# Two-phase feed-forward kernel with chunked attention: q and k of the first eight pairs loaded in 256-byte runs and turned on TensorE

## The reference

```python
scores = q_c @ k_c.T / 8 ; attn = softmax(scores) ; x = attn @ v_c      # per head and 64-row chunk
x = rows of 8 heads x 64 = 512 ; xn = x / rms(x) * rms_g
h = silu(xn @ w_gate) * (xn @ w_val)                                     # 512 -> 1536
y = h @ w_out                                                            # 1536 -> 512
u = y @ w_in2 ; g = u * relu6(u + 3) / 6 ; out = g @ w_out2              # 512 -> 2048 -> 512
```

## Time and profile before

| | |
|---|---|
| median of 3 runs (lowest to highest) | 1726.42 us (1720.36 to 1731.27) |
| profiled execution: time, span | 1721.54 us, 1719.7 us |
| TensorE busy, mean granted clock | 1653.0 us (96%), 0.979 |
| VectorE, ScalarE, GpSimd busy | 1047.3, 869.6, 753.0 us |
| transposed probabilities of pair 6; first product of A | 56.9; 61.51 us |
| first product of phases B, C, D | 711.55, 980.93, 1337.92 us |
| idle of TensorE before products at 874.25 (B), 1028.60 (C) | 0.78, 1.30 us |

### The profile page before, as it was taken

How to read it: one execution, slowest core, us unless ns; L and a number is a source line. 1 busy time by engine, 2 the same in 40 slices (tenths; PEclk the granted TensorE clock), 3 DMA queues, 4 the chain that set the end, 5 groups by cost and what they waited for, 6 DMA issues and landing times.

```text
span 1719.7 us, 29694 instructions
## 1 busy us (share of the span) xinstructions
PE 1653.0 (96%) x11325; PEld 1606.1 (93%) x11330; DVE 1047.3 (61%) x1413; ACT 869.6 (51%) x1361; POOL 753.0 (44%) x711
## 2 busy tenths in 40 slices
PE   6898999999999999999999999999999999999996
PEld 4787988999999999999999999999999999999996
DVE  3877778767755555565554786665666855444442
ACT  3556666664544444454444555554555643433441
POOL 6443434437786665411220467777775510110011
PEclk6899999999999999999999999999999999999998
DMA  9675667635466555788889866557649966666672
GB/s 156 135 183 140 162 156 177 162 106 177 150 234 210 200 201 187 273 284 291 307 305 326 290 232 220 207 182 257 224 169 312 385 212 196 208 216 203 203 219 74
DMA packets 340509, 366.87 MB, mean 213 GB/s; under 512 B 196112, under 2 KB 305424, under 8 KB 337168
## 3 DMA queue, kind: packets, MB, share of 16 engines
q1 hardware_dynamic: 327184, 330.10, 60.9%
q0 software_dynamic: 8832, 34.35, 6.2%
q10 hardware_dynamic: 4352, 0.53, 0.2%
HBM read 200.80 MB, written 164.10 MB: 212 GB/s over the span
## 4 chain that ended last, share of the span: by engine, by line
PE 76%; DVE 4%; DMA 3%; issue 3%; ACT 2%; POOL 2%; DVEq 0%; POOLq 0%; ACTq 0%; SPq 0%
PE bx L861 12%; PE by L861 12%; PE by L863 12%; PE by L862 12%; PE bx L863 12%; PE bx L862 12%; DMA hl_b<-h_scratch 2%; PE att L803 1%; DVE tx L1372 1%; PE att L831 1%; PE att L906 1%; DMA h_scratch<-ht 1%; PE att L840 1%; DMA wr<-wd_scratch 1%; DVE vb L1415 0%
## 5 line engine op out<-in xcount | busy, mean ns | idle before, releaser
L861 PE MATMUL bx<-tx,wr 128*128 128x384 f32 x840 | 287.8, 343 | 9.0 <-ACT gb L1053 3.9
L861 PE MATMUL by<-tx,wr 128*128 128x384 f32 x840 | 288.4, 343 | 5.2 <-DVE ub L1394 4.6
L863 PE MATMUL by<-tx,wr 128*128 128x384 f32 x840 | 282.1, 336 | 0.0
L862 PE MATMUL by<-tx,wr 128*128 128x384 f32 x840 | 281.9, 336 | 0.0
L863 PE MATMUL bx<-tx,wr 128*128 128x384 f32 x840 | 281.8, 335 | 0.0
L862 PE MATMUL bx<-tx,wr 128*128 128x384 f32 x840 | 281.7, 335 | 0.0
L1420 DVE TENSOR_TENSOR hl_d<-hl_d 128x1536 fp32r<-128x1536 f32 x84 | 146.5, 1776 | 88.4 <-ACT hl_d L1129 88.4
L1420 DVE TENSOR_TENSOR hl_b<-hl_b 128x1152 fp32r<-128x1152 f32 x84 | 118.1, 1421 | 106.1 <-ACT hl_b L1129 105.4
L1723 POOL DMA_DIRECT2D out_dram<-row x72 | 37.6, 528 | 309.0 <-ACT row L1171 301.1
L861 PEld LDWEIGHTS bx<-tx,wr 128*128 128x128 f32 x840 | 158.4, 189 | 13.7 <-issue 4.2
L861 PEld LDWEIGHTS by<-tx,wr 128*128 128x128 f32 x840 | 158.5, 189 | 10.8 <-DVE ub L1394 3.7
(11 more groups left out here) (164 smaller groups left out, 3845.1 us busy)
## 6 DMA issues: line engine op xcount, KB each, us to landing
hl_d<-u_scratch SPq DMA_DIRECT2D x84, 768.0 KB, 4.4
hl_b<-h_scratch SPq DMA_DIRECT2D x84, 576.0 KB, 5.5
u_scratch<-ut SPq DMA_DIRECT2D x48, 576.0 KB, 3.6
h_scratch<-ht SPq DMA_DIRECT2D x36, 576.0 KB, 3.7
u_scratch<-ub SPq DMA_DIRECT2D x96, 192.0 KB, 2.9
u_scratch<-ub SPq DMA_DIRECT2D x48, 384.0 KB, 2.9
h_scratch<-vb SPq DMA_DIRECT2D x72, 192.0 KB, 3.3
h_scratch<-vb SPq DMA_DIRECT2D x36, 384.0 KB, 3.3
```

Source lines behind the costliest of these rows:

```text
L861: pe.matmul(dst, w_hi, m_hi, start=start, stop=False, skip_group_check=not opens)
L862: pe.matmul(dst, w_hi, m_lo, start=False, stop=False, skip_group_check=not opens)
L863: return pe.matmul(dst, w_lo, m_hi, start=False, stop=stop, skip_group_check=not opens)
```

## The change

It has three parts.

1. q and k of pairs 0 to 7 are loaded as they lie, in 256-byte runs (one head of one row), two DMAs of 128 KB each for q and for k of a pair: q on SP, k of pairs 0 to 3 on ScalarE's queue, the others on SP. TensorE turns them (`turn_qk`, eight 128x128 transposes of a pair into the bank pair in which the pair's scores will lie), VectorE copies q out (`copy_q`), ScalarE k (`copy_k`). The later pairs stay as they were. The dummy products are placed anew (24, 4 and 4 instead of 18, 2 and one a pair), and GpSimd waits for k of pair 0 before the first load of v and for k of pair 1 before the first raw weights. The weight work of ScalarE and GpSimd in the prologue moves to later pairs; `sums(2)` comes last.
2. The normed rows have two buffers (`xn`, `xn_b`), so that scaling pair n waits for the transposes of pair n-2, no longer n-1.
3. The splits in place, the weight blocks and the units are placed anew: the first half of phase B is split one slot group later and the third moves into phase B; of the splits of phase C one moves to slots 0 and 2 of step 42 and the others to slots 7 and 9, and 9 and 12; block 4 is loaded before GpSimd's last sums of phase A, blocks 5 and 6 wait for one and two products of phase B; unit 22 moves into phase B, and the units there come every 2.5 products instead of every 3.

The core of the diff, without its context lines:

```diff
@@ -108,10 +108,11 @@
-    FIRST_PAIRS = (range(0, 1), range(1, 2), range(2, 4), range(4, 6), range(6, 8))
-    qk_first = [at(f"qk_first{i}", [P, 2, len(FIRST_PAIRS[i]) * D], F32, U0 + (8192, 12288, 16384, 24576, 32768)[i]) for i in range(5)]
+    NQ = 8
+    qk_first = at("qk_first", [P, NQ, 2, D], F32, U0 + 8192)
+    xn_b = at("xn_b", [P, D + 1], F32, U0 + 67584)

@@ -183,8 +184,10 @@
-    q_loaded_first = [sem(f"q_loaded_first{i}") for i in range(5)]
-    k_loaded_first = [sem(f"k_loaded_first{i}") for i in range(5)]
+    q_loaded_first = [sem(f"q_loaded_first{n}") for n in range(NQ)]
+    k_loaded_first = [sem(f"k_loaded_first{n}") for n in range(NQ)]
+    q_turned = sem("q_turned")
+    k_turned = sem("k_turned")

@@ -449,7 +448,7 @@
-    RAW_AT = {6: (14, 9), 7: (14, 10), 8: (16, 11), 9: (16, 13), 10: (18, 11), 11: (18, 13), 12: (19, 12), 13: (20, 2), 23: (34, 13)}
+    RAW_AT = {6: (14, 9), 7: (14, 10), 8: (16, 11), 9: (16, 13), 10: (18, 11), 11: (18, 13), 12: (19, 12), 13: (20, 2), 22: (34, 0)}

@@ -459,7 +458,7 @@
-    U_B = 22
+    U_B = 21

@@ -476,15 +475,15 @@
-        return [u for u in range(U_B + 1, UEND) if 3 * (u - U_B) + after == g]
-    SPLIT_AT = {(0, 0): ((34, 8), (34, 9)), (0, 1): ((34, 10), (34, 11)), (0, 2): ((35, 9), (35, 10)),
-                (0, 3): ((36, 0), (36, 0)), (0, 4): ((36, 1), (36, 1)), (0, 5): ((36, 2), (36, 2)), (0, 6): ((36, 3), (36, 3)),
+        return [u for u in range(U_B + 1, UEND) if 5 * (u - U_B) // 2 + after == g]
+    SPLIT_AT = {(0, 0): ((34, 7), (34, 9)), (0, 1): ((34, 9), (34, 11)), (0, 2): ((35, 7), (35, 9)),
+                (0, 3): ((36, 0), (36, 0)), (0, 4): ((36, 2), (36, 2)), (0, 5): ((36, 3), (36, 3)), (0, 6): ((36, 4), (36, 4)),
-                (1, 2): ((42, 8), (42, 9)), (1, 3): ((42, 10), (42, 11)), (1, 4): ((43, 8), (43, 9)), (1, 5): ((43, 10), (43, 11)),
-                (1, 6): ((44, 8), (44, 9)), (1, 7): ((44, 10), (44, 11)),
-                (2, 0): ((63, 8), (63, 9)), (2, 1): ((64, 8), (64, 9)), (2, 2): ((66, 0), (66, 0)), (2, 3): ((66, 1), (66, 1)),
+                (1, 2): ((42, 0), (42, 2)), (1, 3): ((42, 7), (42, 9)), (1, 4): ((42, 9), (42, 12)), (1, 5): ((43, 7), (43, 9)),
+                (1, 6): ((43, 9), (43, 12)), (1, 7): ((44, 7), (44, 9)),
+                (2, 0): ((63, 7), (63, 9)), (2, 1): ((64, 7), (64, 9)), (2, 2): ((66, 0), (66, 0)), (2, 3): ((66, 1), (66, 1)),

@@ -514,16 +513,12 @@
-        def load_first(i, src, which, loaded):
-            t, p = tp_of(FIRST_PAIRS[i].start)
-            pairs = len(FIRST_PAIRS[i])
-            for piece in range(8):
-                g, b = piece // 2, piece % 2
-                e, hf = g // 2, g % 2
-                by_parity = src[2 * p:2 * (p + pairs)].rearrange("c (j e) (n t) d -> e n t (c j) d", e=2, t=TB)
-                sp.dma_start(qk_first[i][g * TB:(g + 1) * TB, which, :].rearrange("t (m b d) -> t b m d", b=CH // TB, d=TB)[:, b],
-                             by_parity[e, t * (CH // TB) + b][:, :, hf * TB:(hf + 1) * TB]).then_inc(loaded[i], 16)
+        def load_first(n, src, which, loaded):
+            t, p = tp_of(n)
+            for c in range(2):
+                sp.dma_start(qk_first[c * CH:(c + 1) * CH, n, which, :].rearrange("t (h d) -> t h d", d=DH),
+                             src[2 * p + c, :, t * CH:(t + 1) * CH, :].rearrange("h t d -> t h d")).then_inc(loaded[n], 16)

@@ -657,10 +652,10 @@
-        for i in range(5):
-            load_first(i, q, 0, q_loaded_first)
-            if i > 1:
-                load_first(i, k, 1, k_loaded_first)
+        for n in range(NQ):
+            load_first(n, q, 0, q_loaded_first)
+            if n > 3:
+                load_first(n, k, 1, k_loaded_first)

@@ -779,6 +774,14 @@
+    def rows_at(n):
+        return xn_b if n < NG and n % 2 == 1 else xn
+    def turn_bank(n):
+        return bx[:, 0:2] if n % 2 == 1 else att[:, SB:SB + 2]

@@ -804,10 +807,24 @@
+        def turn_qk(n):
+            if n == 0:
+                pe.wait_ge(consts_ready, 2)
+            if n > 1:
+                pe.wait_ge(probsT_copied, n - 1)
+            for i, loaded, done in ((0, q_loaded_first, q_turned), (1, k_loaded_first, k_turned)):
+                pe.wait_ge(loaded[n], 32)
+                by_batch = turn_bank(n)[:, i, :].rearrange("p (c j t) -> p j c t", c=2, j=HJ)
+                for j in range(HJ):
+                    tr = pe.transpose(by_batch[:, j], qk_first[:, n, i, j * P:(j + 1) * P], ident[:, :])
+                tr.then_inc(done, 1)
-                pe.wait_ge(consts_ready, 6)
+                pe.wait_ge(consts_ready, 7)

@@ -864,6 +881,9 @@
+            if m == 0 and st == 0 and o < 2:
+                pe.wait_ge(*((q_transposed, NQ), (k_transposed, NQ))[o])

@@ -912,22 +932,20 @@
-        keep_busy(18)
+        keep_busy(24)
+        turn_qk(0)
+        keep_busy(4)
-        keep_busy(2)
+        turn_qk(1)
+        keep_busy(4)
-            if n < 2 or n == S_FIRST - 1:
+            if n < S_FIRST:
+                scores(n + 1)
+                turn_qk(n + 2)
-                keep_busy(1)
-                scores(n + 1)
-            elif n < S_FIRST:
-                scores(n + 1)
-                attend(n)
-                keep_busy(1)

@@ -978,16 +996,17 @@
-        def load_first_k(i):
-            t, p = tp_of(FIRST_PAIRS[i].start)
-            pairs = len(FIRST_PAIRS[i])
-            for piece in range(8):
-                g, b = piece // 2, piece % 2
-                e, hf = g // 2, g % 2
-                by_parity = k[2 * p:2 * (p + pairs)].rearrange("c (j e) (n t) d -> e n t (c j) d", e=2, t=TB)
-                act.dma_start(qk_first[i][g * TB:(g + 1) * TB, 1, :].rearrange("t (m b d) -> t b m d", b=CH // TB, d=TB)[:, b],
-                              by_parity[e, t * (CH // TB) + b][:, :, hf * TB:(hf + 1) * TB]).then_inc(k_loaded_first[i], 16)
+        def load_first_k(n):
+            t, p = tp_of(n)
+            for c in range(2):
+                act.dma_start(qk_first[c * CH:(c + 1) * CH, n, 1, :].rearrange("t (h d) -> t h d", d=DH),
+                              k[2 * p + c, :, t * CH:(t + 1) * CH, :].rearrange("h t d -> t h d")).then_inc(k_loaded_first[n], 16)
+        def copy_k(n):
+            act.wait_ge(k_turned, n + 1)
+            act.activation(qkT[:, 1, :], turn_bank(n)[:, 1, :], ACT.Copy).then_inc(k_transposed, 1)

@@ -1171,23 +1190,24 @@
-        load_first_k(0)
-        load_first_k(1)
-        act.wait_ge(consts_ready, 6)
+        for n in range(4):
+            load_first_k(n)
+        act.wait_ge(consts_ready, 7)
+        copy_k(0)
+            copy_k(n + 1)
-            if n == 0:
-                weight_hi(0, 0)
-                weight_hi(0, 1)
-                weight_hi(1, n - 2)
+                weight_hi(0, n - 2)
+            if n in (4, 5):
+                weight_hi(1, n - 4)

@@ -1233,9 +1253,8 @@
-                if m == B0 - 1 and slot in (7, 10, 13):
-                    hh = (7, 10, 13).index(slot)
-                    half_hi(0, 0, hh // 2, hh % 2)
+                if m == B0 - 1 and slot in (9, 12):
+                    half_hi(0, 0, 0, (9, 12).index(slot))

@@ -1245,6 +1264,7 @@
+                    half_hi(0, 0, 1, 0)

@@ -1330,6 +1350,11 @@
+        def copy_q(n):
+            dve.wait_ge(q_turned, n + 1)
+            dve.tensor_copy(qkT[:, 0, :], turn_bank(n)[:, 0, :]).then_inc(q_transposed, 1)

@@ -1344,9 +1369,9 @@
-            if n > 0:
-                dve.wait_ge(x_transposed, n)
-            dve.tensor_tensor(by_parity(xn[:, 0:D]), o[:, :, :, 0:DH], row_recip[:, :, :].unsqueeze(3).to_broadcast([P, 2, HJ, DH]), ALU.mult).then_inc(attn_scaled, 1)
+            if n > 1:
+                dve.wait_ge(x_transposed, n - 1 if n <= NG else n)
+            dve.tensor_tensor(by_parity(rows_at(n)[:, 0:D]), o[:, :, :, 0:DH], row_recip[:, :, :].unsqueeze(3).to_broadcast([P, 2, HJ, DH]), ALU.mult).then_inc(attn_scaled, 1)

@@ -1454,16 +1479,13 @@
-        transpose_qk(0)
+        copy_q(0)
-            if n % 2 == 1 or n == S_FIRST:
-                scale_attention(n - 1)
-            transpose_qk(n + 1)
+            copy_q(n + 1)
-            if n in (2, 4):
+            if n > 0:

@@ -1517,9 +1539,8 @@
-                if m == B0 - 1 and slot in (8, 11, 13):
-                    hh = (8, 11, 13).index(slot)
-                    half_lo(0, 0, hh // 2, hh % 2)
+                if m == B0 - 1 and slot in (11, 13):
+                    half_lo(0, 0, 0, (11, 13).index(slot))

@@ -1530,6 +1551,7 @@
+                    half_lo(0, 0, 1, 0)

@@ -1723,39 +1745,41 @@
-        load_raw(0)
-        for const, value in ((half[:, :], 0.5), (minus_half[:, :], -0.5), (xn[:, D:D + 1], (EPS_RMS * D) ** 0.5)):
+        for const, value in ((half[:, :], 0.5), (minus_half[:, :], -0.5), (xn[:, D:D + 1], (EPS_RMS * D) ** 0.5), (xn_b[:, D:D + 1], (EPS_RMS * D) ** 0.5)):
+        pool.wait_ge(k_loaded_first[0], 32)
+        pool.wait_ge(k_loaded_first[1], 32)
+        load_raw(0)
+        load_first_v(1)
```

(35 more changed lines are left out.)

## The result

The changed kernel takes 1712.1 us (median of 11 runs, 1708.2 to 1720.8) where the kernel before takes 1723.6 beside it: a ratio of 0.9937, 95% interval 0.9918 to 0.9956, so 10.9 us (8 to 14) are gained where 26 were forecast. A second set of runs (`after_b`) gave 0.9942 (0.9919 to 0.9964). The profiled execution took 1711.4 us, span 1709.6, 10.1 less than the span before, and it splits by the first product of each phase. "Mark" is the product right behind the x transposes of pair 6, the tenth of phase A, at which TensorE has done the same work in all kernels.

The account below looks back on a forecast made before the run. Loads in 128-byte packets and half-clock TensorE were taken to bound the prologue. Gains 14 (prologue) + 3 (step 0) + 8.4 (passage) + 1.7 (C) - 1 (B) = 26.1 us gave 1700 us against the median 1726.4, range 1688 to 1718.

Parts of the forecast that it names:

- the likeliest case: Whole kernel: the forecast as it stands, 1694 to 1705 us, chance 0.47.
- Passage, B and C: Phase changes: passage from A to B gains 4.2 and 4.2 us, C gains 1.7, B is charged 1.
- The next late thing: Phase B: load of half 6, held on SP by stores of the sums, is late next, about 6 us earlier than now.
- The slower case: Phase B becomes bound by transfers through SP's wait before each of 12 raw loads: 1735 us, chance 0.05.
- the pace of the loop and its start: Prologue: scores 0 at about 10.6, probabilities of pairs 0 and 1 at 14.6 and 18.6, then 4.8 us a pair.
- loads stop being the bound: Prologue: a pair's q and k need 2.2 us of the engines, less than half of a pair's time.
- the term for the work between the pairs: Prologue: GpSimd's weight work between the powers adds 1 us in all.
- they cost nothing: Prologue: the two waits added on GpSimd cost nothing unless k lands after 8 us.
- I take the full clock: Prologue: TensorE stays at full clock, idling some 0.7 of 4.8 us a pair; the half-clock rival, 1722 us, had 0.14.
- step 0: First step of phase A: gains 3 of the 4.2 us lost to half clock, bounds 0 and 4.2.
- half of it arrives: Rival: clock falls for a third of the prologue, powers wait longer, or landing binds the passage; 1705 to 1712, chance 0.28.
- the loads stay the bound: Rival, prologue: 256-byte packets at 17.5 ns, 7 pairs at 6 us, first product at 56; 1708 us, chance 0.06.

Follow-up runs that it names:

- p_tables: Kernel before with only the new places of splits, weight blocks, units and first halves at the phase changes; prologue as before: 1712.2 us, 0.9946 of the kernel before.
- n_gate: m_dum with the raw weights of unit 0 behind the first power too, weight work a pair later, ScalarE's unit 1 parts behind the last norm: 1710.7 us, 0.9941.
- f_fill: Changed kernel with VectorE's split of the first operand behind the last early pair's scores instead of ahead: 0.9943 of the kernel before.
- g3: g2 with the last early pair's power and norm ahead of unit 2's weight load, GpSimd's split and ScalarE's early operand part: 0.9942 of the kernel before.
- m_dum: m_all with dummy products: 8 ahead of pair 3's turn, 2 a pair, 12 at the end: 1707.8 us, 0.9920, and again 1706.5 us, 0.9922.
- c_clock: Changed kernel with added dummies only: 18 ahead of pair 3's turn, 2 a pair, 12 ahead of the sixth's and the last x transposes: 1709.4 us, 0.9920.
- g2: n_gate with unit 0's raw weights loaded once q of pair 3 is there, sums and splits a pair earlier: 0.9924 of the kernel before.
- g2_nod: g2 without dummies except those of the start: 0.9953 of the kernel before; 1717.2 us against g2's 1712.3 on one chip.
- t_dum: p_tables with dummies in TensorE's idle time of the prologue, q and k still by VectorE in 128-byte runs: 0.9951 of the kernel before.
- s_sums2: Changed kernel with GpSimd's sums of unit 2 ahead of the early x sums instead of behind all x sums: 0.9942 of the kernel before.
- p_prologue: Changed kernel with the phase changes' tables, blocks and halves as before, so only the prologue's part: 1719.0 us, 0.9984 of the kernel before.
- m_all: Changed kernel with two GpSimd loads behind powers, unit 1 sums later, first operand's split behind the scores, unit 2 parts three slots later: 1708.1 us, 0.9935.
- l_pure: Changed kernel with two GpSimd loads (unit 1 raw weights, third group's v, 1 MB) issued behind the first power: 0.9945 of the kernel before.
- after: The changed kernel itself, first set of runs and its profile: 1712.1 us, 0.9937 of the kernel before.
- l_loads: l_pure with GpSimd's and ScalarE's weight work also moved to later pairs: 0.9955 of the kernel before.

## Why the prediction was right and wrong

The time lies in the range (1712 in 1688 to 1718), but the gain is less than half of the forecast's, and the likeliest case was not the one that came. By the 1% bound it is "within 1%", which had 0.25.

*Right: the phase changes.* Passage, B and C were given 9.1 us together (8.4 and 1.7 less 1); `p_tables` measured 9.3 (6 to 13), and the profile shows 4.1, 2.6 and 2.2 by phase, less 1.8 in D. The places are less sure than the sum: `p_tables` has 3.2, 1.6, 2.2 and -0.3 there. The next late thing was the half held on SP, as named. The slower case, raw loads in phase B, did not show: its largest wait after the passage is 0.88.

*Right: the pace of the loop and its start.* Scores 0, pair 0 and pair 1 came within 0.8 us of the forecast; a pair takes 4.61 at full clock where nothing is late, and `n_gate` ran pairs 3 to 6 near that pace.

*Wrong: "loads stop being the bound".* This is the step that failed for the first product. It compared q and k's 2.2 us of the engines a pair with the pair's time and left out GpSimd's 2.5 MB, which now all go out between 6.4 and 15.2 us (v of the second and third groups of pairs went at 22.5 and 29.1 before, at 10.4 and 13.5 after). That made q of pair 3 late by 4.26 us and, with the clock, pair 2's probabilities by some 5.5. I had priced the packets from stretches in which nothing else moved, and not asked who shares the engines. With fewer loads ahead of it, q lands some 3 us sooner (`n_gate`).

*Wrong: the term for the work between the pairs.* The other 4 us of the 9.4 by which the first product was late stand ahead of pairs 5 and 6. For GpSimd's weight work I had added 1 us, but 18.6 and five pairs of 4.8 are 42.6, so the sum does not hold it; its sums of unit 1 cost 1.34 at one place. VectorE's split of the first operand was in no term: it is the 2.69 ahead of pair 6 (`f_fill`: 0.34 with it moved).

*Wrong: "they cost nothing"*, of the two waits added on GpSimd. k of pair 1 landed at 8.85, past the 8 us that I had set, and TensorE waited 0.92 us for the first v at 17.47. Queued behind the waits are not only v and the norms, which I named, but the raw weights, and behind those GpSimd's sums and splits of two units and the x sums. With the loads early, q is late; with the loads late (`n_gate`, `g3`), that line is late. With first products at 48.91 and 50.58, near the forecast's, the marks of these two are 75.38 and 76.08, and their totals are the changed kernel's. That this step takes the rest of the gain is argued from these rows and not shown: no run takes the two waits out, and `m_dum`, with unit 0's raw weights where the changed kernel has them, has no wait on the second operand and its mark at 72.3. The forecast ended its count at the first product; once that is early, the prologue ends with the second operand.

*Wrong by size: the clock.* "I take the full clock" held where TensorE was not waiting, so the reasoning on the loop was right; the waits above brought half clock for 7 us in one profile of the changed kernel and 18 in the other. The dummies that hold it up are worth 3 to 5 us (`c_clock`, `g2` against `g2_nod`; the intervals overlap), and nothing in the prologue before (`t_dum`).

*Wrong by sign: step 0.* The 3 us became -1.7, since GpSimd's sums of unit 2 came behind the x sums: ScalarE stood 3.15 us for them, TensorE 2.49, with half clock behind it from 67 to 71. I had named this move as a delay of ScalarE's parts by 2 us and counted it as 1.2 off the gain. Without it (`s_sums2`) TensorE's wait is 1.08, behind VectorE and ScalarE, but the total is the same; why is open.

*The rivals.* Both that were to take the gain came true together: "half of it arrives" (the clock falls for a third, 1705 to 1712) and "the loads stay the bound" (first product at 56, 1708); it was at 56.88. I gave them 0.28 and 0.06 as if they excluded each other, though one wait brings both. That 56.88 is so near 56 is luck: the rival had seven pairs at 6 us, the profile has one long wait and pairs of 4.6 to 7.7.

Open: phase D takes 1.8 us more after the change, in the second profile too, but only 0.3 more in `p_tables` and 0.5 in `p_prologue`. TensorE's waits in it are 0.9 more in sum; the rest has no row.

## What to carry to other kernels

When a chain of loads gets faster, list every other transfer that is in flight in the same stretch, by queue and packet size: small packets that shared the engines with large ones advanced one for one here (241 to 243), not byte for byte. Before counting a prologue's gain to its first product, follow each engine that feeds the second and third, above all one that has to wait for the loads that were just put back. Where TensorE was at half clock in these prologues, it had waited: find the wait, then ask what the clock adds.

## What the runs showed that I had not expected

One queue with packets of 3.3 KB (0.79 MB in 243) held another with 256-byte packets to 60 packets a microsecond, in every kernel profiled with these loads (16 to 20 us, GpSimd's first: `p_prologue` 245 to 246, `m_all` 250 to 246, `l_pure` 249 to 248), against some 480 a microsecond (1932 in 20 to 24 us of `m_all`) once the first was nearly done (63 packets).

The mean granted clock of one kernel varies from run to run, 0.982 to 0.990 in the changed one, and its time with it: 1720.8 us at 0.982, 1708.2 at 0.988, on a line fitted to its 11 runs 1.2 us for each 0.001 (correlation 0.8). After waits of 4.26, 2.16, 2.47 and 4.41 us for pair 3 the clock stayed at half for 7, 11, 14 and 46 us (`after`, `l_loads`, `l_pure`, `m_all`), so the length does not follow the wait. A single profile of a prologue is one draw: the changed kernel's first product was at 56.88 in one and 60.95 in the other.
